# Attention, rational layer and gated layer on one core: other sizes for the first loads, and a new way and place for the norms of q

## What is computed

```python
qn = q / (norm(q, axis=1) + 1e-6)          # one norm per column, over the 6016 rows
kn = k / (norm(k, axis=1) + 1e-6)
s  = kn.T @ qn / tau                       # 256 x 256
a  = softmax(s, axis=-1)
x  = v @ a                                 # 6016 x 256
h  = x @ w_in                              # 6016 x 2048
g  = (a0 + a1 h + a2 h^2 + a3 h^3) / (1 + |b0||h| + |b1| h^2 + 1e-6)
y  = g @ w_out                             # 6016 x 256
out = (sigmoid(y @ w_gate) * (y @ w_val)) @ w_out2
```

## Time and profile before

| | us |
|---|---|
| runs before: median of 3 | 1206.06 |
| lowest, highest | 1205.66, 1206.26 |
| the profiled execution | 1205.5 |
| its span in the trace | 1203.7 |
| TensorE busy in the span | 1191.9 |
| VectorE busy | 1064.7 |
| ScalarE busy | 881.3 |
| GpSimd busy | 253.8 |

### The profile page before, as it was taken

One profiled execution on the slowest core, in us unless ns is written; L12 is line 12 of the kernel. 1 busy time (PEld: TensorE's weight loads), 2 busy tenths in 40 slices (PEclk: granted clock), 3 DMA queues, 4 the chain that ended last, 5 costly groups with the idle time before them and its releaser, 6 DMA issues.

```text
span 1203.7 us, 19532 instructions
## 1 busy us (share of the span) xinstructions
PE 1191.9 (99%) x6772; PEld 1165.5 (97%) x6772; DVE 1064.7 (88%) x1369; ACT 881.3 (73%) x1267; POOL 253.8 (21%) x152
## 2 busy tenths in 40 slices
PE   9998999999999999999999999999999999999998
PEld 8876999999999999999999999999999999999998
DVE  7799999899999989999998999899898989989843
ACT  6898778677777868777786877778687777768632
POOL 0432212112121212212121211212121221212110
PEclk9999999999999999999999999999999999999999
DMA  9820000000000000000000000000000000000000
GB/s 368 300 66 13 1 14 14 13 13 0 13 13 13 13 13 13 0 13 13 13 13 13 13 0 13 13 13 13 13 13 0 13 13 13 13 0 13 0 14 14
DMA packets 15866, 33.81 MB, mean 28 GB/s; under 512 B 1382, under 2 KB 6246, under 8 KB 15846
## 3 DMA queue, kind: packets, MB, share of 16 engines
q1 hardware_dynamic: 14982, 32.51, 7.5%
q10 hardware_dynamic: 864, 1.05, 0.3%
HBM read 27.39 MB, written 6.16 MB: 28 GB/s over the span
## 4 chain that ended last, share of the span: by engine, by line
PE 90%; DVE 5%; DMA 2%; SPq 1%; issue 1%; ACT 1%; DVEq 0%; ACTq 0%
PE ps L905 17%; PE ps L903 17%; PE ps L904 17%; PE ps L1017 7%; PE ps L1018 7%; PE ps L1019 7%; PE ps L1056 5%; PE ps L1058 5%; PE ps L1057 5%; DMA kq<-in_q 2%; PE ps L917 1%; SPq L340 1%; SPq L342 1%; PE ps L940 1%; DVE work L875 0%
## 5 line engine op out<-in xcount | busy, mean ns | idle before, releaser
L453 POOL TENSOR_TENSOR g_parts<-work,g_parts 128x752 fp32r<-128x752 f32 x120 | 218.7, 1822 | 814.4 <-ACT g_parts L634 814.4
L624 ACT ACTIVATE work<-ps,neg_a 128x752 f32<-128x752 f32 x120 | 117.6, 980 | 143.5 <-PE ps L905 82.1
L903 PE MATMUL ps<-v_hi,m_hi 128*128 128x376 f32 x512 | 174.1, 340 | 1.2 <-DVE work L862 1.0
L905 PE MATMUL ps<-v_hi,m_lo 128*128 128x376 f32 x512 | 171.5, 335 | 0.0
L904 PE MATMUL ps<-v_lo,m_hi 128*128 128x376 f32 x512 | 170.4, 333 | 0.0
L1017 PE MATMUL ps<-g_parts,w_hi 128*128 128x376 f32 x480 | 160.7, 335 | 0.0
L1018 PE MATMUL ps<-g_parts,w_hi 128*128 128x376 f32 x480 | 160.0, 333 | 0.0
L1019 PE MATMUL ps<-g_parts,w_lo 128*128 128x376 f32 x480 | 159.4, 332 | 0.0
L748 DVE TENSOR_TENSOR work<-work,ps 128x376 f32<-128x376 f32 x192 | 103.7, 540 | 52.6 <-PE ps L905 39.8
L856 DVE TENSOR_TENSOR work<-work,ps 128x752 f32<-128x752 f32 x120 | 112.0, 934 | 37.7 <-ACT work L627 36.0
L660 ACT ACTIVATE work<-work,consts 128x752 f32<-128x752 int32 x118 | 108.4, 918 | 38.7 <-DVE work L875 38.7
(11 more groups left out here) (131 smaller groups left out, 2862.8 us busy)
## 6 DMA issues: line engine op xcount, KB each, us to landing
work<-in_v SPq DMA_DIRECT2D x16, 376.0 KB, 2.9
out<-work SPq DMA_DIRECT2D x15, 376.0 KB, 2.3
kq<-in_k SPq DMA_DIRECT2D x9, 512.0 KB, 13.2
kq<-in_q SPq DMA_DIRECT2D x9, 512.0 KB, 15.5
before<-in_moe_w_out SPq DMA_DIRECT2D x5, 512.0 KB, 12.6
before<-in_moe_w_in SPq DMA_DIRECT2D x8, 256.0 KB, 7.1
before<-in_moe_w_gate SPq DMA_DIRECT2D x2, 512.0 KB, 9.5
before<-in_moe_w_val SPq DMA_DIRECT2D x2, 512.0 KB, 6.7
```

The costliest lines, as they stand in the source:

```text
L453: nc.gpsimd.tensor_tensor(g_lo[n], g[n], as_f32(g_hi[n]), ALU.subtract).then_inc(g_lo_ready, 1)
L624: nc.scalar.activation(poly[n], h, ACT.Identity, scale=neg_a[:, 3:4], bias=neg_a[:, 2:3])
L903: nc.tensor.matmul(dst, l_hi, r_hi, start=(begins and n == 0), stop=False)
L905: last = nc.tensor.matmul(dst, l_lo, r_hi, start=False, stop=(ends and n == len(parts) - 1))
```

## The change

Four things. The loads take six times 1 tile, once 2, once 3 and nine times 4, seventeen in all; the first six q loads on ScalarE's queue now carry six tiles instead of eight, and the broadcast of the coefficients keeps its tile. q's sums come out as two columns, like k's, and ScalarE takes one root of all four; VectorE adds q's guard and inverts two columns, multiplies the identity with each (`q_diag`), and TensorE spreads them to a row on all partitions by a product of ones with the diagonals (`spread_q`); VectorE copies that row from PSUM to SBUF. The norms stand before tile 37 instead of 33, the spread before tile 40. The rest of the program is as it was.

```diff
-    KQ_SIZES = [1] * 4 + [2] * 2 + [4] * ((NT - 8) // 4)
-    KQ_SIZES[6:6] = [NT - sum(KQ_SIZES)]
+    KQ_SIZES = [1] * 6 + [2] + [4] * ((NT - 8) // 4)
+    KQ_SIZES[7:7] = [NT - sum(KQ_SIZES)]
-    COEF_SPREAD_BEFORE = 9
+    COEF_SPREAD_BEFORE = 10
-    NORMS_AT, TURN_AT = NT - 14, NT - 2
+    NORMS_AT, SPREAD_AT, TURN_AT = NT - 10, NT - 7, NT - 2
...
-            nc.scalar.activation(q_inv, ps_qnorm, ACT.Sqrt).then_inc(norms_squared, 1)
-            nc.scalar.activation(k_norm, ps_knorm, ACT.Sqrt).then_inc(norms_squared, 1)
+            nc.scalar.activation(norms_kq, ps_norms, ACT.Sqrt).then_inc(norms_squared, 1)
             act.wait_ge(norms_squared, 1)
-            nc.scalar.activation(q_inv, q_inv, ACT.Identity, bias=norm_guard).then_inc(norms_rooted, 1)
-            act.wait_ge(norms_squared, 2)
             act.wait_ge(coefs_ready, 1)
-            nc.scalar.activation(k_norm, k_norm, ACT.Identity, scale=neg_tau,
+            nc.scalar.activation(k_norm, norms_kq[:, 0:CC], ACT.Identity, scale=neg_tau,
                                  bias=neg_tau_guard).then_inc(norms_rooted, 1)
...
+            dve.wait_ge(norms_squared, 1)
+            link(nc.vector.tensor_scalar(q_inv, q_inv, 1e-6, None, ALU.add))
+            link(nc.vector.reciprocal(q_inv, q_inv))
+            dve.wait_ge(ident_ready, 1)
+            for c in range(CC):
+                nc.vector.tensor_scalar(q_diag[:, c, :], ident[:], q_inv[:, c:c + 1], None,
+                                        ALU.mult).then_inc(q_diag_ready, 1)
             dve.wait_ge(norms_rooted, 1)
-            link(nc.vector.reciprocal(q_inv, q_inv))
-            dve.wait_ge(norms_rooted, 2)
             link(nc.vector.reciprocal(k_inv, k_norm))
             for c in range(CC):
                 if c == 0:
+                    dve.wait_ge(q_row_ready, 1)
+                    link(nc.vector.tensor_copy(q_row, ps_qrow))
                     dve.wait_ge(first_scores, 1)
...
-                                                    in1=q_inv, op0=ALU.mult, op1=ALU.mult))
+                                                    in1=q_row, op0=ALU.mult, op1=ALU.mult))
...
                 pe.wait_ge(summed, 2 * (len(KQ_CHUNKS) + 3))
-                for c in range(CC):
-                    nc.tensor.matmul(ps_knorm[:, c:c + 1], k_acc[:, 0, c * P:(c + 1) * P], ones[:, 0:1],
-                                     start=True, stop=True)
-                nc.tensor.matmul(ps_qnorm, ones[:], q_acc[:, 0, :], start=True,
-                                 stop=True).then_inc(norms_summed, 1)
+                for n in range(2 * CC):
+                    acc, c = (k_acc, q_acc)[n // CC], n % CC
+                    last = nc.tensor.matmul(ps_norms[:, n:n + 1], acc[:, 0, c * P:(c + 1) * P], ones[:, 0:1],
+                                            start=True, stop=True)
+                last.then_inc(norms_summed, 1)
+
+            def spread_q():
+
+                pe.wait_ge(q_diag_ready, CC)
+                nc.tensor.matmul(ps_qrow, ones[:], q_diag.rearrange("p a b -> p (a b)"), start=True,
+                                 stop=True).then_inc(q_row_ready, 1)
...
                 if late == NORMS_AT:
                     norms()
+                if late == SPREAD_AT:
+                    spread_q()
                 if late == TURN_AT:
                     turn(0)
                 score(late, 1).then_inc(kq_multiplied, 1)
```

More of the change, by code:

```diff
@@ L163, in attention_rational_gated_kernel @@
         assert 4 * KQ_W <= 6 * PW
-        q_inv = region(6 * PW, (C,))
+        q_row = region(6 * PW, (C,))
+        q_diag = region(6 * PW + 5 * C, (CC, P))
         att = region(6 * PW + C, (CC, C))
@@ L176, in attention_rational_gated_kernel @@
         neg_min, row_sum, row_inv = small[:, 6:8], small[:, 8:10], small[:, 10:12]
+        norms_kq, q_inv = small[:, 12:16], small[:, 14:16]
         consts = sb("consts", [P, 7])
@@ L189, in attention_rational_gated_kernel @@
         ps_kq = ps[:, 0:2, 0:C]
-        ps_knorm, ps_qnorm = ps[:, 2, 0:CC], ps[:, 3, 0:C]
+        ps_norms, ps_qrow = ps[:, 2, 0:2 * CC], ps[:, 5, 0:C]
         ps_coef = ps[:, 4, 0:7]
@@ L204, in attention_rational_gated_kernel @@
         norms_summed, norms_rooted, small_step = sem("norms_summed"), sem("norms_rooted"), sem("small_step")
+        q_diag_ready, q_row_ready = sem("q_diag_ready"), sem("q_row_ready")
         scores_ready, exps_ready, row_inv_ready = sem("scores_ready"), sem("exps_ready"), sem("row_inv_ready")
```

## The result

The changed kernel takes 1212.06 us (median of 7 runs, 1207.61 to 1213.09), the one before 1205.75 on the same chip (7 runs, 1205.42 to 1206.26): a ratio of 1.0049, 95% interval 1.0039 to 1.0058. It is 6.3 us slower where 0.4 us faster was forecast. One of the seven executions, 1207.61, stands apart from the six between 1211.25 and 1213.09.

A forecast was written before the change was run, and what follows sets the result against it. TensorE was taken as the bound, busy 1191.9 of 1203.7 us. Gain 0.33 without the early gain, 0.47 capped with all of it; 0.4 taken: 1206.06 - 0.4 = 1205.7 us, range 1204.8 to 1206.6.

The forecast's parts named there:

- part 2: Chain from norms to first turn: diagonal products 0.57 us together, turn at 46.90 instead of 47.23, gain 0.33 us.
- Rival (c): Diagonal products and small steps before them wait for a GpSimd instruction, up to 2.33 us: +1.9 us (1208.0); chance 0.07.
- its doubled form: Two VectorE instructions near the diagonal products held by GpSimd instead of one: +4.2 us (1210.3).
- TensorE's wait of 1.10 us at the norms: Before the norms' first weight load: four more products first remove this wait; net on TensorE -0.65 us.
- From the spread to the turn 2.78: TensorE's spread starts at 44.12; copy, product, reduction and exponential follow, and the first turn can start at 46.90.
- without an early gain: Case where the new loads win nothing before the norms: first turn at 46.90, gain 0.33 us.
- part 3: Opening loads, six of one tile: early waits for q shrink, worth 0 to 0.45 us on the way to the norms.
- The early holes: TensorE's waits of 0.74 and 0.40 us before tiles 4-5 and 6-7, expected to shrink; at most 1.14 us.
- the slack of 0.45 at tiles 11 and 27: Margin between q's landing and TensorE's arrival there; any early load gain beyond 0.45 us is given back.
- the part on what is late next: Behind the second turn, a weight half's load landing at 50.95 lets at most 0.47 us of gain pass.
- rival (a): The weight landing at 50.95 is no cap, loads land earlier: gain 0.78 to 1.1 us, 1205.0 to 1205.3; chance 0.15.

The follow-up runs named there:

- GpSimd later: The changed kernel with GpSimd's four subtractions held back until both diagonal products are done: 1206.25 us against 1205.56 for the kernel before.
- the kernel with PSUM inputs: The changed kernel with identity and q's roots put in PSUM, read there by the addition and both diagonal products: 1205.46 us against 1205.39 for the kernel before.
- TensorE kept busy: The changed kernel with 18 spare products of 128 columns ahead of TensorE's wait for the diagonal: 1210.35 us, ratio 1.0042 to the kernel before.
- the new loads alone: The kernel before with only the new load sizes (six single tiles first): 1205.06 us against 1205.33.
- the one-product kernel: The changed kernel with PSUM inputs, but the second diagonal product reads the identity from SBUF: median 1206.01 us, ratio 1.0011 to the kernel before.
- the kernel with only one product in the changed form: The changed kernel with addition and first diagonal product reading two SBUF inputs, second product as changed: 1211.94 us, ratio 1.0047 to the kernel before.

## Why the prediction was wrong

**The step that failed** is in part 2: "They lie between the 0.15 of 128x4 and the 0.42 of a 128x256 reduction or copy; halfway is 0.285, two are 0.57". The rows that I interpolated between are of another kind. The 128x4 instruction reads PSUM, and ran with GpSimd idle; the copy reads PSUM too; and the reduction, within SBUF, took its 0.42 in the midst of GpSimd's work. None of them can show a hold; the diagonal products are held. By themselves they take 0.48 us for both (GpSimd later), as good as estimated; beside GpSimd 4.42. The same holds for the addition: 0.17 by itself, 0.68 beside GpSimd, though it has two elements a partition. The length of a hold doesn't follow the size of the held instruction but what is left of GpSimd's 2.35 us: beside GpSimd the addition on two columns took from 0.60 to 1.70 us over the profiles with SBUF inputs.

**Rival (c) was the right mechanism**, with a chance of 0.07. I counted the reduction at 45.93 against it, which couldn't speak to it, and its doubled form gave 4.2 us. What I left out of its price is the second effect: a hole of over 4 us on TensorE is not only its own length. Put together: the spread starts at 44.22 in the kernel with PSUM inputs and at 48.63 in the changed one, which are the holds, 4.4 us. From there to the turn it is 2.9 us with the clock at 1.00 (both with PSUM inputs and with TensorE kept busy) and 4.8 in the changed kernel, which is the clock, 1.9. With 47.12 being 0.1 under the 47.23 of before, that is 6.2 in all.

The Trainium skill ("SBUF — State Buffer", SBUF: two separate sides) states the rule that I should have put in the place of the interpolation: VectorE and GpSimd share one pair of SBUF ports as an exclusive lock, whoever starts first has it for the whole instruction, and a VectorE instruction wants it in a two-port mode or, against a GpSimd instruction that reads SBUF as this one does, with two SBUF inputs. The traces agree: 2.13 and 2.38 us in the changed form, 4.55 for both with two inputs, 0.61 for both with a PSUM input. That the one-input products were in a two-port mode no trace shows by itself; what the runs show is which forms were held.

**What else of the prediction stood.** TensorE's wait of 1.10 us at the norms went, and they started at 41.84 (41.4 to 41.9 was said). The four one-column products took 1.00 us, not 0.90 (41.77 to 42.77 with PSUM inputs). From the spread to the turn 2.78 was said; with PSUM inputs it was 2.90 (44.22 to 47.12). The turn was forecast for 46.90 without an early gain and came at 47.12, with one root more. The gain of part 3 on the way to the norms was nil in the changed kernel, inside the 0 to 0.45: 41.84 against 40.17 + 1.71 = 41.88. The early holes weren't filled but moved: TensorE now waited for q 0.51 us before the pair of tiles 6-7 and 0.33 before the load of tile 8, and reached tile 11 at about 14.2, where 14.28 had been worked out for the kernel before. So the slack of 0.45 at tiles 11 and 27 was never used, and no wait came there. Without the holds the time was 1205.46 for a forecast of 1205.7; against the kernel before on its own chip that is +0.07, where -0.4 was forecast, and both lie within what can be told. In its profile 0.26 us arrives at the split of the attention tile (51.77 for 52.03) and 0.2 at the end (a span of 1203.5 for 1203.7).

**What else failed** is the part on what is late next, without effect on the time here. "That load is bound by the transfer backlog, not by this chain" made a fixed point of 50.95. The weight is issued some 5.1 to 5.2 us after the last q has landed and lands 10 us later, so it moves with the landings: to 50.41 with the new loads alone and 50.46 with PSUM inputs, as rival (a) had it (its gain of 0.78 to 1.1 us didn't come), and to 51.68 in the kernel with GpSimd later, where the last q was late and the split waited 0.52 us for it.

The odd execution of 1207.61 has a mean clock of 1.000, the six others 0.997 or 0.998. It fits a run in which one product found GpSimd's gap and the hole stayed short; the one-product kernel has two such groups. It was not traced.

## What to carry to other kernels

Before pricing a new VectorE instruction by the nearest row, ask where its inputs lie and whether GpSimd is running: within SBUF, as a `tensor_scalar` with one input or with two inputs, it can cost most of a GpSimd instruction, be it two elements wide. Inputs in PSUM removed this here. And price a hole on TensorE with what the products behind it cost at the lower clock.

## What was unexpected of the hardware

Two consecutive products don't share one gap of a GpSimd stream without pauses: GpSimd's next instruction starts before the second product does (46.16 against 46.20 in the changed kernel, and 0.05 to 0.11 us ahead in the five other profiles with two held products), and the second pays a full instruction. VectorE's small reciprocals and its reduction, SBUF to SBUF with one input, were not held: 0.17 us at 43.36 with PSUM inputs, in the midst of GpSimd's instruction of 41.64 to 43.99, and 0.42 at 45.93 in the kernel before. The granted clock didn't always fall within the hole: in the kernel with only one product in the changed form it read 1.00 over the hole, 44.57 to 49.70, and up to 50, and fell behind it, with the products already running again (stretches of that kernel):

```profile
49.00:50.00 1.00, 0.30 (x1) 0.30 (x2) 0.72 (x2) 0.00 (x0) 0.56 (x1) 1.00 1.05 387
50.00:51.00 1.00, 1.00 (x4) 0.85 (x3) 0.43 (x2) 0.00 (x0) 0.00 (x0) 0.62 1.04 383
51.00:52.00 1.00, 1.00 (x4) 0.75 (x3) 0.89 (x2) 0.04 (x1) 0.00 (x0) 0.50 1.06 389
```

And the last q landed at different times from execution to execution, read from the square that it released: between 35.07 and 36.50 us over the ten profiles with the new load sizes, between 35.90 and 37.12 over the four with the old ones. Either spread is three times the 0.4 us that was forecast, or more.
